# Each head's scores by its own matmul over 64 rows of the array, with r unpadded, and a ring of two level buffers of two PSUM banks each

## The reference

```python
for t in range(S):
    cur = np.einsum('bhd,bhe->bhde', u[None] * kt, vt)
    y[:, :, t] = np.einsum('bhd,bhde->bhe', rt, state + cur)
    state = wt[:, :, :, None] * state + np.einsum('bhd,bhe->bhde', kt, vt)
# x: y by token (2 x 768 tokens, 384 features)
x = x + relu(layer_norm(x) * g_ln @ w_ch1) @ w_ch2           # 384 -> 1536 -> 384
u, v = halves of relu(x @ w_in)                              # 384 -> 1024
out = (u * (w_spatial @ normalized(v) + b_spatial)) @ w_out  # 512 -> 384
```

## Time and profile before

| | us |
|---|---|
| median of 3 runs | 484.99 |
| lowest, highest | 484.53, 485.33 |
| profiled execution, span from first to last instruction | 483.2 |
| busy: TensorE, its loads | 438.5, 413.5 |
| busy: DVE, ACT, GpSimd | 282.0, 209.3, 150.2 |

### The profile page before, as it was taken

One profiled execution on the slowest core, in us unless ns is written; L12 is line 12 of the kernel. 1 busy time (PEld: TensorE's weight loads), 2 busy tenths in 40 slices (PEclk: granted clock), 3 DMA queues, 4 the chain that ended last, 5 costly groups with the idle time before them and its releaser, 6 DMA issues.

```text
span 483.2 us, 7994 instructions
## 1 busy us (share of the span) xinstructions
PE 438.5 (91%) x2724; PEld 413.5 (86%) x2724; DVE 282.0 (58%) x600; ACT 209.3 (43%) x486; POOL 150.2 (31%) x234
## 2 busy tenths in 40 slices
PE   3688779877877799999999999999999999999997
PEld 3587669776767689999999999999999998898997
DVE  6999999999999997124422432333241684413120
ACT  4787667667776673322212321332221752211211
POOL 6586666668776673600000000100010530000000
PEclk9999997799999999999999999999999999999999
DMA  7434432334432112200000000000410110010102
GB/s 222 139 79 118 116 99 72 85 92 123 124 85 72 50 36 68 65 1 0 1 0 1 1 1 1 0 1 0 152 44 1 33 34 2 0 50 1 50 1 97
DMA packets 26540, 25.59 MB, mean 53 GB/s; under 512 B 1666, under 2 KB 21890, under 8 KB 26500
## 3 DMA queue, kind: packets, MB, share of 16 engines
q1 hardware_dynamic: 26500, 25.08, 17.7%
HBM read 22.72 MB, written 2.36 MB: 52 GB/s over the span
## 4 chain that ended last, share of the span: by engine, by line
PE 63%; DVE 7%; issue 2%; ACT 1%; POOL 0%; DVEq 0%; ACTq 0%
PE bank L1122 20%; PE bank L1124 19%; PE bank L1123 19%; DVE score L773 3%; DVE wtot L731 2%; PE bank L1100 1%; PE bank L1207 1%; PE bank L1028 1%; DVE rin L750 1%; DVE sdec L804 1%; DVE ku L783 0%; PE bank L1069 0%; PE bank L1071 0%; PE bank L1070 0%; DVE state L820 0%
## 5 line engine op out<-in xcount | busy, mean ns | idle before, releaser
L1028 PE MATMUL bank<-rz,k 128*128 128x128 f32 x576 | 85.4, 295 | 28.9 <-DVE score L773 15.2
L1028 PEld LDWEIGHTS bank<-rz,k 128*128 128x128 f32 x576 | 74.3, 202 | 38.0 <-issue 36.7
L572 ACT COPY rz<-rin 64x256 f32<-64x256 f32 x144 | 58.7, 408 | 42.7 <-DVE rin L750 36.6
L773 DVE COPY_PREDICATED score<-msk,bank 128x512 f32<-128x512 int32 x84 | 74.0, 881 | 0.9
L511 POOL TENSOR_TENSOR vrstd<-vmv,half 128x1 f32<-128x1 f32 x12 | 7.7, 643 | 156.5 <-DVE vmv L974 156.5
L494 POOL TENSOR_TENSOR k<-k,wtot 128x256 f32<-128x256 f32 x60 | 42.8, 714 | 1.6
L466 POOL TENSOR_TENSOR k<-kin,ucol 128x128 f32<-128x128 f32 (+2 forms) x72 | 22.4, 311 | 54.5 <-ACT k L597 53.3
L887 DVE SCALAR_TENSOR_TENSOR h11l<-bank,h11h 128x384 fp32r<-128x384 f32 x24 | 13.4, 557 | 37.4 <-ACT h11h L660 37.4
L750 DVE TENSOR_TENSOR rin<-rin,wtot 128x256 f32<-128x256 f32 x60 | 32.8, 547 | 3.0 <-ACT rz L572 2.7
L660 ACT ACTIVATE h10h<-bank 128x384 fp32r<-128x384 f32 x24 | 11.8, 490 | 51.2 <-PE bank L1124 51.2
L887 DVE SCALAR_TENSOR_TENSOR h10l<-bank,h10h 128x384 fp32r<-128x384 f32 x24 | 13.4, 557 | 34.4 <-ACT h10h L660 34.4
(11 more groups left out here) (158 smaller groups left out, 1162.7 us busy)
## 6 DMA issues: line engine op xcount, KB each, us to landing
stage<-in_w SPq DMA_DIRECT2D x12, 384.0 KB, 3.3
vin<-in_v SPq DMA_DIRECT2D x12, 288.0 KB, 2.8
rin<-in_rT SPq DMA_DIRECT2D x12, 256.0 KB, 4.4
win<-in_wT SPq DMA_DIRECT2D x12, 256.0 KB, 3.6
kin<-in_kT SPq DMA_DIRECT2D x12, 256.0 KB, 4.4
out<-ob SPq DMA_DIRECT2D x12, 192.0 KB, 1.9
stage<-in_w_in SPq DMA_DIRECT2D x4, 384.0 KB, 3.2
x<-in_w_sp SPq DMA_DIRECT2D x4, 384.0 KB, 5.0
```

What stands on the lines that cost most here:

```text
L572: last = sc.copy(dst, src[lo:hi, :, :, :])
L773: ve.copy_predicated(dst, mb, src).then_inc(scores_placed, 1)
L1028: mm = te.matmul(b_level[n % 3][:, a * P:(a + 1) * P], kk[:, a, :], rz[l][:, a, :, :].rearrange("p e t -> p (e t)"), start=True, stop=True)
```

## The change

`rz` becomes `rc[l]`, pair x 64 columns, with both heads on their own partitions and no zeros; ACT fills it by one copy of 128 partitions (`take_right`). The seven memsets go. Each pair's matmul is replaced by two, one for each head: weights are the 64 partitions of k that hold the head (128 columns), the moving side the same 64 partitions of `rc` (64 columns), and head e writes to bank e of a pair of banks. A level buffer has now two banks, half of each used (4 pairs x 64 columns), and `b_level` is a ring of two: level n waits for the selection of level n - 2. `score` is laid out head-in-pair x pair x token to fit, and the selection reads both banks by one instruction. With four banks for levels, y has one bank in place of two: the attention products of tile i wait until y of tile i - 1 has been taken to x. The banks of the dense blocks are dealt out anew; the first early product waits for the turned k (`kt_ready`) in place of a selection.

```diff
         kc = {c: place(f"k_{c}", [P, NPR, P]) for c in LEVELS[1:] + [P]}
-        rz = [place(f"rz{l}", [P, NPR, 2, P // 2]) for l in range(NL)]
-        score = [place(f"score{q}", [P, H, P]) for q in range(2)]
+        rc = [place(f"rc{l}", [P, NPR, P // 2]) for l in range(NL)]
+        score = [place(f"score{q}", [P, 2, NPR, P]) for q in range(2)]
         kt = [place(f"kt{q}", [P, NPR, P]) for q in range(2)]
...
         assert max(attention_end, ff_end) <= nc.sbuf_usable_end
-        bank = [ctx.enter_context(nc.psum_tensor(f"bank{q}", [P, BANK], F32)) for q in range(8)]
-        b_level = bank[0:3]
-        b_ktr, b_ds, b_y = bank[3], bank[4], [bank[5], bank[6]]
-        b_f1 = bank[0:2]
-        b_acc = bank[2:5]
+        b_level = [ctx.enter_context(nc.psum_tensor(f"levels{q}", [P, 2, BANK], F32)) for q in range(2)]
+        bank = [b_level[q // 2][:, q % 2, :] for q in range(4)]
+        bank += [ctx.enter_context(nc.psum_tensor(f"bank{q}", [P, BANK], F32)) for q in range(4, 8)]
+        b_ktr, b_ds, b_y = bank[4], bank[5], bank[6]
+        b_f1 = [bank[4], bank[0]]
+        b_acc = bank[1:4]
         b_vu = bank[5:7]
         b_turn = bank[7]
         b_own = b_ds[0:1, D:D + H]
         def b_tr(step, g, a):
-            return bank[a] if (step, g) == ("X2T", NG - 1) and a < 2 else b_turn
+            return b_f1[a] if (step, g) == ("X2T", NG - 1) and a < 2 else b_turn
         w1s = [ffw[:, e * W1C:(e + 1) * W1C] for e in range(2)]
...
                 gp.tensor_tensor(dst[:, i:i + 1], src[:, i, 1:2], half[:, :], ALU.pow).then_inc(std_ready, 1)
-            for l in (0, 2, 4, 6):
-                gp.memset(rz[l][:, :, :, :], 0.0).then_inc(zeroed_by_pool, 1)
-            gp.memset(score[1][:, :, :], 0.0).then_inc(scores_zeroed, 1)
+            gp.memset(score[1][:, :, :, :], 0.0).then_inc(scores_zeroed, 1)
             with_u(0, 0)
             gp.memset(half[:, :], -0.5)
-            gp.memset(state[:, :, :], 0.0).then_inc(zeroed_by_pool, 1)
+            gp.memset(state[:, :, :], 0.0).then_inc(state_zeroed, 1)
             k_left(0, 0)
...
             sc = nc.scalar
-            def pad(i, l):
+            def take_right(i, l):
                 q = i % 2
...
                     act.wait_ge(level_done, NL * (i - 1) + l + 1)
-                elif l % 2 == 0:
-                    act.wait_ge(zeroed_by_pool, l // 2 + 1)
-                else:
-                    act.wait_ge(zeroed_by_vector, l // 2 + 1)
-                for e, (lo, hi) in enumerate(HALF):
-                    dst = rz[l][lo:hi, :, e, :]
-                    if l:
-                        dst = dst.rearrange("p a (m c) -> p a m c", c=LEVELS[l])
-                        last = sc.copy(dst, src[lo:hi, :, :, :])
-                    else:
-                        last = sc.copy(dst, src[lo:hi, :, :])
-                last.then_inc(padded_r_ready if l else padded_r0_ready, 1)
+                dst = rc[l][:, :, :]
+                if l:
+                    dst = dst.rearrange("p a (m c) -> p a m c", c=LEVELS[l])
+                sc.copy(dst, src).then_inc(right_r_ready if l else right_r0_ready, 1)
             def k_pairs(i):
...
                 act.wait_ge(y_done, i + 1)
-                sc.copy(x[:, i, :], b_y[i % 2][:, 0:D]).then_inc(x_ready, 1)
+                sc.copy(x[:, i, :], b_y[:, 0:D]).then_inc(x_ready, 1)
             def split_vn(i):
                 b, c = i // CH, i % CH
                 act.wait_ge(vn_ready, i + 1)
                 sc.copy(vns[b][0][:, c * DH:(c + 1) * DH], vn[:, i, :]).then_inc(vn_hi_ready, 1)
-            pad(0, 0)
+            take_right(0, 0)
             k_pairs(0)
             k_right(0, 0)
             for i in range(NT):
                 for l in range(1, NL):
-                    pad(i, l)
+                    take_right(i, l)
                     if l == 5 and i + 1 < NT:
-                        pad(i + 1, 0)
+                        take_right(i + 1, 0)
                     k_right(i, l)
...
                     dve.wait_ge(y_done, i - 1)
-                src = b_level[(NL * i + l) % 3][:, :].rearrange("p (h t) -> p h t", h=H)
+                src = b_level[(NL * i + l) % 2][:, :, 0:BANK // 2].rearrange("p e (a t) -> p e a t", a=NPR)
                 mk = msk[:, l, :]
+                heads = score[q][:, :, :, :].rearrange("p e a t -> p (e a) t")
                 if l == 0:
-                    dst = score[q][:, :, :].rearrange("p h (m two) -> p h m two", two=2)[:, :, :, 1]
+                    dst = heads.rearrange("p h (m two) -> p h m two", two=2)[:, :, :, 1]
                     mb = mk[:, None, :].to_broadcast([P, H, P // 2])
                 else:
                     c = LEVELS[l]
-                    dst = halves(score[q][:, :, :], c)[1]
-                    src = src.rearrange("p h (m c) -> p h m c", c=c)
+                    dst = halves(heads, c)[1]
                     mb = mk.rearrange("p (m c) -> p m c", c=c)[:, None, :, :].to_broadcast([P, H, P // (2 * c), c])
-                if l == NL - 1:
-                    dst, src, mb = dst[:, :, 0, :], src[:, :, 0, :], mb[:, :, 0, :]
+                    if l == NL - 1:
+                        dst, mb = dst[:, :, 0, :], mb[:, :, 0, :]
                 ve.copy_predicated(dst, mb, src).then_inc(scores_placed, 1)
...
                     dve.wait_ge(y_done, i - 1)
-                ve.tensor_copy(score[i % 2][0:1, :, 0], b_own).then_inc(own_in_score, 1)
+                ve.tensor_copy(score[i % 2][0:1, :, :, 0], b_own.rearrange("p (a e) -> p e a", e=2)).then_inc(own_in_score, 1)
             def decay_state(i):
...
                 elif i == 0:
-                    dve.wait_ge(zeroed_by_pool, 5)
+                    dve.wait_ge(state_zeroed, 1)
                 dve.wait_ge(gain_done, carried(i))
...
                 return [(i + 1, l)] if i + 1 < NT else []
-            for l in (1, 3, 5):
-                ve.memset(rz[l][:, :, :, :], 0.0).then_inc(zeroed_by_vector, 1)
-            ve.memset(score[0][:, :, :], 0.0).then_inc(scores_zeroed, 1)
+            ve.memset(score[0][:, :, :, :], 0.0).then_inc(scores_zeroed, 1)
             ve.memset(ones_c[:, :], 1.0).then_inc(own_parts_set, 1)
...
                     kk = kc[LEVELS[l]]
-                if n >= 3:
-                    te.wait_ge(scores_placed, n - 2)
+                if n >= 2:
+                    te.wait_ge(scores_placed, n - 1)
                 for a in range(NPR):
-                    mm = te.matmul(b_level[n % 3][:, a * P:(a + 1) * P], kk[:, a, :],
-                                   rz[l][:, a, :, :].rearrange("p e t -> p (e t)"), start=True, stop=True)
+                    for e, (lo, hi) in enumerate(HALF):
+                        mm = te.matmul(b_level[n % 2][:, e, a * P // 2:(a + 1) * P // 2], kk[lo:hi, a, :],
+                                       rc[l][lo:hi, a, :], start=True, stop=True)
                 mm.then_inc(level_done, 1)
...
                     te.wait_ge(own_in_score, i + 1)
-                    if i >= 2:
-                        te.wait_ge(x_ready, i - 1)
-                o = b_y[q][:, 2 * HD * a:2 * HD * (a + 1)]
+                    if i >= 1:
+                        te.wait_ge(x_ready, i)
+                o = b_y[:, 2 * HD * a:2 * HD * (a + 1)]
                 if not first(i):
                     te.matmul(o, rin[i % 4][:, a, :], state[:, a, :], start=True, stop=False)
-                te.matmul(o, score[q][:, 2 * a, :], vin[q][:, a, 0:2 * HD], start=first(i), stop=False)
-                mm = te.matmul(o, score[q][:, 2 * a + 1, :], vin[q][:, a, HD:3 * HD], start=False, stop=True)
+                te.matmul(o, score[q][:, 0, a, :], vin[q][:, a, 0:2 * HD], start=first(i), stop=False)
+                mm = te.matmul(o, score[q][:, 1, a, :], vin[q][:, a, HD:3 * HD], start=False, stop=True)
                 if a == NPR - 1:
...
                     split_waits(te, W1C // STAGE - 1)
-                if n < 2:
-                    te.wait_ge(scores_placed, NL * NT - 2 + n)
+                if n == 0:
+                    te.wait_ge(kt_ready, carried(NT - 1))
+                if n == 1:
+                    te.wait_ge(scores_placed, NL * NT - 1)
                 if f == 0:
```

More of the change, by code:

```diff
@@ L198, in rwkv_moe_kernel @@
         chunk_in_sbuf = [sem(f"chunk_in_sbuf{q}") for q in range(2 + X_SLOTS)]
-        zeroed_by_pool = sem("zeroed_by_pool")
-        zeroed_by_vector = sem("zeroed_by_vector")
+        state_zeroed = sem("state_zeroed")
         scores_zeroed = sem("scores_zeroed")
@@ L214, in rwkv_moe_kernel @@
         r_ready = sem("r_ready")
-        padded_r0_ready = sem("padded_r0_ready")
-        padded_r_ready = sem("padded_r_ready")
+        right_r0_ready = sem("right_r0_ready")
+        right_r_ready = sem("right_r_ready")
         own_uk_ready = sem("own_uk_ready")
@@ L281, in run_ends, with right_r @@
             return z[:, :, :, side]
-        def padded(eng, i, l):
+        def right_r(eng, i, l):
             if l == 0:
```

(8 more changed lines are left out.)

## The result

The changed kernel takes 564.97 us (564.87 to 565.11, 4 runs) against 485.0 of the kernel before: ratio 1.165, 95% interval 1.163 to 1.167. That is 80.0 us slower. The forecast was 484.8 and the range ended at 528.

A forecast was written before the change was run, and what follows sets the result against it. DVE was taken to bound the recurrence, TensorE the products behind it. Terms -1.7 + 0.4 + 0.7 + 0.4 = -0.2 us on a 483.2 us span, plus 1.8 around it, gave 484.8 us; range 480 to 528.

The forecast's parts named there:

- The bound before: Whole kernel: DVE bounds the recurrence up to about 185 us, TensorE the products behind it; other engines run ahead and wait.
- The matmuls: Levels on TensorE: 16 loads side by side on the two halves, a level still about 1.1 us, cost 0.
- 64 moving columns in place of 128 save nothing: Levels on TensorE: the weight load of 128 columns sets the pace, not the width of the moving side.
- Rival D: Recurrence: the half-full array stands at 1.2 GHz over much of the stage; +30 over half of it, 515 us; chance 0.05.
- Rival B: Levels on TensorE: 64-row loads queue, TensorE becomes the bound; +38, 523 us (512 to 545); chance 0.30.
- Rival C: TensorE: switches between 64-row and 128-row work cost more than measured, +9.6 at 0.4 each, 494 us (489 to 500); chance 0.15.
- The ring: Level buffers, ring of two: +0.7 us (0 to 3) inside the stage and +0.4 at its end.
- One bank for y costs 0: Attention output: one bank in place of two costs 0, as y's next write comes two levels after tile i's end.
- ACT: Copies of r: one in place of two takes 34 us off ACT; DVE waits less, -1.7 us (2.3 at most).
- Zeroing: Seven memsets on GpSimd and DVE go; both engines then wait for loads anyhow: cost 0, gain up to 1.6 us.
- The second stage: Products on TensorE after the recurrence: length kept, about 298 us from the first product on.
- The range of A: The forecast case, loads side by side and DVE still the bound: 480.5 to 489 us; chance 0.45.

The follow-up runs named there:

- the third experiment: The changed kernel with each 64-row matmul streaming its 64 columns twice (128 columns), the second copy into an unused part of the bank: 493.35 us.
- the warm start: The changed kernel with six matmuls of 128 x 512 on ones ahead of the first level, to raise the clock once: 565.3 us.
- heads-apart kernel: The changed kernel with a level's eight matmuls reordered, the four of head 0 first, then the four of head 1: 629.0 us.
- all of the buffers: The changed kernel with padding, memsets and one 128-row matmul per pair back; ring of two, banks and single y bank kept: 491.17 us.
- the ring alone: The kernel before with two level banks in place of three and the early products' banks dealt out to fit: 490.48 us.
- the late copy of y: The 128-column kernel with ACT's copy of y to x moved behind the next tile's second copies of r and k: 489.14 us.

## Why the prediction was wrong

**The bound before** was read rightly: DVE, with TensorE, ACT and GpSimd waiting. What I left out of that reading is on what the TensorE line rested. It had a stretch at 1.2 GHz in which it was busy 6.53 of 6.6 us; so at the low clock TensorE has nothing left in this stage, and the pace of the stage hung on the high clock.

**The matmuls: the step that failed.** The term that failed is "cost 0" for a level's matmuls. I worked it out at 2.4 GHz alone, with a level at about 1.1 us. That much was right: side by side, 0.97 us for 16 loads (the third experiment and the warm start). But the stage ran at 1.2 GHz, where a level takes 1.97 us and TensorE is busy for 160.0 of 160 us, and the first dense product came 79.2 us late. "64 moving columns in place of 128 save nothing" was true of time and missed what it did to the clock. The Trainium skill's sentence (TensorEngine Tiling (Array Packing), Key Properties) that different tiles load and multiply in parallel held (0.097 us for a load in turn, 0.157 on one half, both at 1.2 GHz). The Trainium skill's rule (TensorE: Matmul & The Clock Gate, LDWEIGHTS) that a load's time goes by columns, not rows, agrees with the recorded length of one load at 1.2 GHz, 325 ns over 64 rows in the heads-apart kernel and 333 over 128 rows in the one with eight matmuls over all rows. The pace of a load with its multiplication doesn't follow it: 0.157 us on one half, 0.214 over all rows.

**Rival D** had the mechanism, the levels at 1.2 GHz, and two sizes wrong. I gave it half of the stage, and it was all of it, which with its own 5 us for a tile would have made +60 in place of +30; and 20 us for a tile of tokens, where the mean is 21.4. The first and the last own term of the kernel before (L1041) and of the kernel after (L1030):

```profile
14.77 0.20 PE L1041 MATMUL bank<-ruk,ones_c 128*1 128x8 f32 x2
...
178.71 0.20 PE L1041 MATMUL bank<-ruk,ones_c 128*1 128x8 f32 x2
```

```profile
17.31 0.20 PE L1030 MATMUL bank<-ruk,ones_c 128*1 128x8 f32 x2
...
252.37 0.20 PE L1030 MATMUL bank<-ruk,ones_c 128*1 128x8 f32 x2
```

Between them lie 11 tiles: (178.71 - 14.77)/11 = 14.9 us each before, (252.37 - 17.31)/11 = 21.4 after (14.8 for the first, which has no attention work, up to 23.4 for later ones). That makes 71.1 of the 79.2 us; 2.5 lie ahead of the first own term and 5.6 behind the last. The 1.4 us over my 20 are within what the changes between 64 and 128 rows cost, some 12 in a tile. From the last load of an attention pair (148.84 + 0.22 = 149.06) to the next level's first (149.56) it is 0.50 in place of 0.215; from the last load of a level (146.13 + 1.79 - 0.33 = 147.59) to the next attention load 0.45. So a change costs 0.24 to 0.29 us more than a plain step, about 3 us in a tile. I gave D 0.05, because its only argument was the half-full array and the rows held no narrow matmul. That chance was far too small: the slow stretch in rows 2 showed a clock that already fell in this stage, and a change that halves what each multiplication streams is the first thing to hold against it. The reason that I gave, a half-full array, was wrong as well: with all rows in use and 64 columns the clock stayed down, and with half of them and 128 columns it rose.

**Rival B** (queued loads) gave the nearest place in the range, but by the wrong mechanism. **Rival C** (a switch at 0.3 us or more) didn't come: the 0.2 us measured at the own term held at 2.4 GHz. In the kernel with 128 columns, an attention load pair starts at 185.50 and the next level at 185.90, 0.3 after its last load in place of 0.11.

**The ring** was charged 1.1 us and costs 5.6. I followed TensorE's queue to DVE's selection and stopped there; that loop has its slack (1.2 us of waits). The queue that I didn't follow is ACT's: the later level delays the attention product, that delays ACT's copy of y, and behind it in ACT's order stand the next tile's r and k, for which DVE waits. "One bank for y costs 0" was right to within 0.7 us: 491.17 with all of the buffers against 490.48 with the ring alone, with overlapping intervals.

**ACT**: 84 copies of r of 412 ns, 33.5 us in all, in place of 168 with 68.8, which are the 34 us that I said. Its busy time falls by more, from 209.3 to 166.1 us; the other 8 us were not followed. With the clock down nothing of it, and so nothing of the term of -1.7 us, reaches the end. With 128 columns and the late copy of y, DVE's waits for ACT's r from 0 to 215 us are 1.2 us against 3.9 before, which is about what the term stood for. **Zeroing** cost 0, as said: DVE's first product starts at 5.06 in place of 4.98 and GpSimd's at 6.74 in place of 6.86. **The second stage** (298.9 against 298.0 us) kept its length, as said.

**The range of A**: its lower end, 480.5, doesn't follow from the bounds that I named, which add up to no less than 481. Nothing rests on it.

What stays open: what exactly in 64 streamed columns keeps the clock down (columns, or their share of the time that loads take) wasn't told apart, the levels' clock was not followed down from a busy stretch at 2.4 GHz, and where the last 2 us of the ring go was not followed to the end.

## What to carry to other kernels

A change that makes matmuls narrower or shorter is to be costed at both clock levels of TensorE: if the kernel has a stretch at 1.2 GHz, look there at what the stage would be if it stayed down, and ask whether the change takes away the streaming that keeps it up. Don't trust the clock column alone; compare the spacing of an instruction that was not changed. When a buffer ring is shortened, follow the delay through every engine's queue, not only through the two engines that share the ring.

## What the runs showed of the hardware

- TensorE can be busy all the time and stay at 1.2 GHz: 166.5 of 168 us in the warm-start kernel at a granted clock of 0.50.
- Adding streamed columns made the kernel faster: 564.97 us with 64, 541.99 with 96, 493.35 with 128, for the same loads and the same useful result.
- At 1.2 GHz a load and its multiplication follow each other by 0.097 us on alternating halves, 0.157 on one half, and 0.214 over all rows; at 2.4 GHz 16 alternating loads take the same 0.97 us as 8 over all rows.
- A granted clock of 1.00 in a row can mean that no change was recorded yet: the changed kernel's whole first stage reads 1.00 and ran at 1.2 GHz; its first record is at 266.7 us.
